# A planner's model of the opening's DMA loads is refitted, and with it the order of every engine's work

## What is computed

```python
out_d = sm_attn(q_d, k_d, v_d)                # q, k, v averaged over groups of 4 tokens
out_up = np.repeat(out_d, 4, axis=2)
mask = np.abs(pos[:, None] - pos[None, :]) < 4
scores = np.where(mask, scale * q @ k.T, -1e9)
out_local = softmax(scores) @ v
x = (out_up + out_local) as [tokens, 512]
h = x @ w_in;  g = s * relu(h)**2 + b;  x = g @ w_out      # layer 1
h = x @ w_in2; g = h - tanh(h);         out = g @ w_out2   # layer 2
```

## Time and profile before

| what | us |
|---|---|
| median of 3 runs | 893.32 |
| lowest, highest | 892.18, 893.84 |
| the profiled execution | 892.53 |
| its span | 890.7 |
| TensorE busy in the span | 876.7 |
| VectorE, ScalarE, GpSimd busy | 592.2, 467.4, 362.7 |

### The profile page before, as it was taken

How to read it: one execution, slowest core, us unless ns; L and a number is a source line. 1 busy time by engine, 2 the same in 40 slices (tenths; PEclk the granted TensorE clock), 3 DMA queues, 4 the chain that set the end, 5 groups by cost and what they waited for, 6 DMA issues and landing times.

```text
span 890.7 us, 15923 instructions
## 1 busy us (share of the span) xinstructions
PE 876.7 (98%) x5956; PEld 824.6 (93%) x5956; DVE 592.2 (66%) x799; ACT 467.4 (52%) x1144; POOL 362.7 (41%) x348
## 2 busy tenths in 40 slices
PE   7999999999999999999999999999999999999997
PEld 6889999999999999999999998988899888998896
DVE  5658599989999999985213377677734447444444
ACT  2899575567545754545565454444533336333332
POOL 5567473966489663433732100022221315212120
PEclk8999999999999999999999999999999999999999
DMA  8971453353333323202102250110601001310012
GB/s 219 277 247 46 120 147 85 106 128 94 97 94 88 88 46 72 71 1 79 56 28 65 80 181 24 27 45 25 189 25 44 29 24 48 95 43 29 24 49 71
DMA packets 57904, 73.57 MB, mean 83 GB/s; under 512 B 19110, under 2 KB 36068, under 8 KB 57828
## 3 DMA queue, kind: packets, MB, share of 16 engines
q1 hardware_dynamic: 56233, 72.12, 29.3%
q10 hardware_dynamic: 1595, 0.43, 0.2%
HBM read 63.10 MB, written 9.44 MB: 81 GB/s over the span
## 4 chain that ended last, share of the span: by engine, by line
PE 92%; DVE 3%; ACT 2%; DMA 1%; issue 1%; SPq 1%; POOL 0%; ACTq 0%; DVEq 0%; POOLq 0%
PE acc L2226 23%; PE hid L2198 22%; PE hid L2263 19%; PE acc L2280 14%; PE pa L2280 7%; PE pa L2156 1%; PE pa L2123 1%; PE pa L1998 1%; DMA dkey<-in_k_dram 1%; PE pa L2140 1%; DVE x2l L1610 1%; PE pa L2169 1%; PE acc L1990 1%; DVE sum L1655 0%; PE hid L2206 0%
## 5 line engine op out<-in xcount | busy, mean ns | idle before, releaser
L1248 POOL TENSOR_TENSOR gl<-relu,gh 128x288 fp32r<-128x288 f32 x128 | 128.3, 1005 | 171.1 <-PE acc L2226 119.5
L2226 PE MATMUL acc<-gh,wbh 128*128 128x288 f32 (+1 forms) x512 | 154.5, 302 | 0.0
L2198 PE MATMUL hid<-xh,wah 128*128 128x288 f32 x512 | 153.5, 301 | 0.3 <-ACT relu L1886 0.2
L2226 PE MATMUL acc<-gl,wbh 128*128 128x288 f32 (+1 forms) x512 | 151.5, 296 | 0.0
L2226 PE MATMUL acc<-gh,wbl 128*128 128x288 f32 (+1 forms) x512 | 151.2, 295 | 0.0
L2198 PE MATMUL hid<-xh,wal 128*128 128x288 f32 x512 | 150.4, 295 | 0.0
L2198 PE MATMUL hid<-xl,wah 128*128 128x288 f32 x484 | 142.0, 294 | 0.0
L1886 ACT ACTIVATE relu<-hid 128x288 f32<-128x288 f32 x128 | 52.3, 408 | 129.9 <-PE hid L2198 107.6
L2263 PE MATMUL hid<-x2h,wqh 128*128 128x384 f32 x336 | 113.2, 337 | 2.4 <-DVE odd L1646 2.4
L2263 PE MATMUL hid<-x2h,wql 128*128 128x384 f32 x336 | 113.2, 337 | 0.0
L2263 PE MATMUL hid<-x2l,wqh 128*128 128x384 f32 x336 | 112.8, 336 | 0.0
(11 more groups left out here) (210 smaller groups left out, 1863.7 us busy)
## 6 DMA issues: line engine op xcount, KB each, us to landing
w2b_raw<-in_moe_w_out_dram SPq DMA_DIRECT2D x24, 512.0 KB, 3.6
kl<-in_k_dram SPq DMA_DIRECT2D x23, 240.0 KB
vl<-in_v_dram SPq DMA_DIRECT2D x23, 240.0 KB
x2T<-ystage SPq DMA_DIRECT2D x8, 576.0 KB, 3.2
own<-in_q_dram SPq DMA_DIRECT2D x11, 384.0 KB
wa_raw<-in_moe_w_in_dram SPq DMA_DIRECT2D x4, 1024.0 KB, 8.8
wb_raw<-in_moe_w_out_dram SPq DMA_DIRECT2D x4, 1024.0 KB, 10.4
x2raw<-x2T SPq DMA_DIRECT2D x10, 384.0 KB, 3.9
```

Source lines behind the costliest of these rows:

```text
L1248: g.tensor_tensor(out=gl[:, turn % LRING1, 0:NS], in0=relu[:, f % 2, :], in1=gh[:, turn % GRING1, 0:NS].bitcast(F32), op=ALU.subtract).the ...
L2198: one = pe.matmul(dst, w[:, group, d, cols], x[:, j % XRING, d, :], start=i == 0, stop=i == 3 * KT - 1)
L2226: one = pe.matmul(acc[:, d, n], w[:, f, cols], g[:, turn % ring, n], start=(f == 0 and p == 0), stop=(f == FT - 1 and p == 2))
```

## The change

Only the planner's model of loads is edited. The modelled pipe is free at 2.0 us instead of 0; data counts as landed 1.5 us after the load leaves the pipe instead of 0.6, for every load of the program; and the sizes of the opening's loads are new. All orders, and the counts of fillers, follow from it. No instruction of the computation, no buffer and no wait is edited.

```diff
+FIRST_PACKET, LANDING = 2.0, 1.5
-        dma_free, emptied, held = 0.0, [0.0, 0.0], set()
+        dma_free, emptied, held = FIRST_PACKET, [0.0, 0.0], set()
                 dma_free = max(dma_free, start + 1.4) + kbytes / 230.0
-                end = dma_free + 0.6
+                end = dma_free + LANDING
-            o.add("SP", 0.6, (2, 2 * g + 3 * i), (kind, g), after, kbytes=620)
+            o.add("SP", 0.6, (2, 2 * g + 3 * i), (kind, g), after, kbytes=690)
-        o.add("SP", 1.6, (0, 0, half, 6), ("load_dense_keys", half), kbytes=330)
-    o.add("ACT", 2.5, (0, 0), ("load_first_queries",), kbytes=330)
-    o.add("SP", 1.6, (0, 0, 1, 6, 1), ("load_last_queries",), kbytes=330)
-    o.add("SP", 3.0, (1, 0, 0), ("load_dense_values",), kbytes=870)
+        o.add("SP", 1.6, (0, 0, half, 6), ("load_dense_keys", half), kbytes=360)
+    o.add("ACT", 2.5, (0, 0), ("load_first_queries",), kbytes=360)
+    o.add("SP", 1.6, (0, 0, 1, 6, 1), ("load_last_queries",), kbytes=360)
+    o.add("SP", 3.0, (1, 0, 0), ("load_dense_values",), kbytes=850)
-    for i, (kind, kbytes) in enumerate((("load_late_keys", 600), ("load_late_queries", 590), ("load_late_values", 870))):
+    for i, (kind, kbytes) in enumerate((("load_late_keys", 730), ("load_late_queries", 730), ("load_late_values", 850))):
-                  kbytes=(240 if b else 200) if n < 6 else 180)
+                  kbytes=(240 if b else 300) if n < 6 else 175)
```

## The result

The changed kernel takes 894.83 us (median of 19 runs, 892.68 to 896.21), the kernel before 892.84 (19 runs, 892.12 to 894.0). The ratio is 1.0019, 95% interval 1.0011 to 1.0026: slower by 0.19%, or 1.7 us (the medians themselves lie 2.0 apart). That is inside the 0.2% which the prediction called no change, but its sign is against the forecast of 891.1, and the interval holds no gain. Its runs also spread over 3.5 us, where those of before, taken with them, spread over 1.9; but 27 runs of the kernel before, taken later with other kernels, spread over 3.8. The profiled execution is 894.57 us, its span 892.8.

A forecast was written before the change was run, and what follows sets the result against it. ScalarE was taken to pace the opening behind the gate, TensorE the rest. Span 890.7 - 2.2 = 888.5, plus 1.8 gives 890.3, plus 0.8 for the median 891.1 us; range 888.9 to 895.3.

The forecast's parts named there:

- What bounds the kernel, and the gate: Opening: `dense_turn` 2 waits for loads until 17.33 us, unchanged; then ScalarE sets the pace to 43.31, TensorE bounds the rest.
- Whether the new model is nearer the trace: Opening's loads: old plan some 4 us early by the gate, new one within 0.7 us everywhere but 1.1 at the last.
- Fillers: TensorE ahead of the gate: 36 fillers for 24 move the first `dense_turn` from 7.5 to 8.1 us, costing nothing.
- VectorE: Opening: `dense_max` 0 goes ahead of the key sums; wins nothing by itself, may cost 0.5 us through `dense_keys` 2.
- ScalarE ahead of the gate: Three `place_columns`, from about 16 us, and `dense_exp` 1 move into ScalarE's idle time before 17.33: 2.73 us of work.
- The gain at `hidden1` (0, 0): End of the opening: 2.2 us sooner, at 41.1, between bounds of 1.7 and 2.73.
- The clock at the gate, priced at nothing: TensorE behind 17.33 us: full clock saves 2 to 3 us of its work, priced at nothing because ScalarE sets the pace.
- The failed step: Behind `hidden1` (0, 0): ScalarE's order nearly unchanged, reshuffles of batches 1 to 3 priced at 0, bounds -1.0 and +2.4 us.
- `load_w1b` 0 lands at 41.6, its first split comes at 42.5, nothing stands.: ScalarE behind `hidden1` (0, 0): weights needed at most 2.2 us sooner still land before their first use, so no wait.
- The slower one: 43 to 100 us: ScalarE bounds, four weight splits ahead of one `activate1` cost 2.1 us, twice 4.2; 895.3 us, chance 0.14.
- Lost on the way: Opening ends sooner, but later steps wait as much or ScalarE idles; gain 0 to 1.2, about 893 us, chance 0.23.
- the one for being wrong: Wrong if the gate moves, line 2198 starts as late as before, or the stretch behind `hidden1` grows by over 2 us.

The follow-up runs named there:

- the first experiment: Changed kernel with the modelled size of the eight w1 loads put back from 690 to 620: 890.29 us, 0.9975 of before.
- the run with the moved split: Kernel before with `w1_high` (0, 0) planned behind `score_exp` (0, 3): 892.05 us without added fillers, 891.36 with 26 more ahead of `dense_turn` 2.

## Why the prediction was wrong

The forecast was 891.1 and faster; the truth is 894.83 and slower by 0.19%.

- **What bounds the kernel, and the gate.** Right: loads stayed, the gate stayed, and nothing but the orders moved.
- **Whether the new model is nearer the trace.** Right, with one slip: the first value stage, planned at 22.2 and traced at 21.41, is 0.8 us off, not within 0.7.
- **Fillers.** The counts 36 and 28 are exact. The first `dense_turn` was to come at 8.1 and came at 7.22: the 36 took 5.78 us in all where 24 had taken 5.16. Their pace goes from some 0.21 us each to 0.12 on the way, and the moment varies from run to run: the same 24 fillers ended at 6.68 us in the kernel before and at 5.86 in the one with the gate filled, and with the same 36 the first `dense_turn` came at 8.27 in the kernel of the first experiment. The profile's granted clock is 1.00 for all of that time and does not show the step. The price of nothing was right: the gate waited for its loads all the same.
- **VectorE.** The order came as worked out. The feared half microsecond for `dense_keys` 2 did not arise: its copy was expected at 18.7 and ran at 18.03.
- **ScalarE ahead of the gate.** Right in mechanism and content (three `place_columns`, `dense_exp` 1), about 1 us sooner than forecast (14.89 against 16).
- **The gain at `hidden1` (0, 0).** 3.37 us, where 2.2 was taken with 2.73 as the upper bound. The stretch from `dense_queries` 2 got 24.68 - 21.67 = 3.0 us shorter (2.6 forecast), and it began 0.36 sooner. The mechanism was right: ScalarE's work there fell by 2.74 us (20.64 to 17.90), and its idle from 4.04 to 3.77. The bound of 2.73 left out the sooner start and the idle.
- **The clock at the gate, priced at nothing.** In the kernel before this is nearly right: full clock there alone moved `hidden1` (0, 0) by nothing and the time by 0.7 us, at the edge of the noise. In the new order the lower clock behind the gate goes with 1.1 us, and taking all fillers away costs 2.4. A price taken from one order was used in another.
- **The failed step: "its steps behind `hidden1` are the same and in nearly the same order, since their ranks decide", priced at 0 with bounds -1.0 and +2.4.** It cost 6.1 us, of which 4.5 are the late split with all that the plan puts in front of it and 1.6 the late load on top. I followed the plan only up to `hidden1` (0, 0), where it gave the right order, and put a phrase in place of the rest. Ranks decide only among steps that can start at the same time; in the plan `w1_high` (0, 1) is held back by the modelled landing of `load_w1b` 0 at 42.7, the splits behind it come later with it, and by then attention steps are ready that pass `w1_high` (4, 0). The kernels that move this one split show it in both directions (-4.5 and +4.1 us). The other part of the same pricing, a reshuffle of batches 1 to 3 at no cost, was right.
- **"`load_w1b` 0 lands at 41.6, its first split comes at 42.5, nothing stands."** Wrong too, since `hidden1` (0, 0) came 1.2 us sooner than forecast and the load 1.2 us later: the split came at about 40.5, the load landed at 42.75, ScalarE stood 2.24 us. Worth 0.7 to 1.9 us, by the measure taken.
- **The rivals.** The slower one had the right engine, the right stretch (43 to 100 us) and nearly the right time (895.3), but the wrong mechanism: splits set ahead of an `activate1`, at 2.1 us each. In truth splits were set too late, and two fifths of the cost, 2.5 us, are the clock, which it did not have. Its condition, over 4.0 us of new idle, was not met: it was 3.6. That its time came out so near is luck. "Lost on the way" (893) was too small and named no place. Of the signs set down, the one for being wrong decided: the stretch behind `hidden1` (0, 0) grew by over 2 us.

Why did a truer model of the loads make a slower order? By the planner's own count nothing was lost: it sees the new order and the one with the split back as equal to within 0.2 us at the end. It does count TensorE's idle around the late split, 5.9 us from `hidden1` (0, 0) up to 60 us against 2.5 with the split back. But in the order with the split back it counts 3.3 us more from 60 to 120 us, where that kernel's trace has 0.6. So it thinks the idle only moved. And it knows no clock, which is the other 2.5 us. What stays open is why the runs of the changed kernel spread over 3.5 us. The clock does not tell them apart: its mean over each run is 0.994 to 0.996 in all 19, 0.996 in the slowest and 0.995 in the fastest.

## What to carry to other kernels

When a planner's input changes, follow its orders past the point where the gain is booked, to the place where the next scarce engine is full, and look at which long steps of the bottleneck engine have moved behind short ones. A gain in the opening brings everything behind it forward against loads that have not moved, so list each load's landing and the new time of its first use before pricing the rest at nothing. Short waits close together can cost more than their sum: here two of 1.3 and 1.4 us with short steps between them were followed by 6.8 us of lower clock.

## What the runs showed of the hardware

- Behind two waits of 1.31 and 1.37 us with short steps between, TensorE went to 1.2 GHz for 6.8 us in the changed kernel, and again in the kernel before with the late split (0.67 from 60 to 70) and in the one with early load and late split. In the changed kernel without fillers, where the same two waits are 0.98 and 1.37, the low stretch lasted 3.4 us (60.2 to 63.6). Single idle times were followed by the same fall: 3.18 us at the gate in the kernel before and 2.39 us in the kernel with early load and late split (0.74 from 17.33 to 24). Filled to 1.11 us, the idle time at the gate of the kernel before was followed by none (1.00 from 17.33 to 24).
- A VectorE instruction that reads two SBUF tiles stands while GpSimd works on two SBUF tiles: a product takes 1.93 us beside GpSimd's subtraction against 0.51 with GpSimd idle. It happened again in the run with the moved split, where GpSimd made two low parts from 39.23 to 41.73; VectorE's and GpSimd's rows of that kernel:

```profile
40.91 1.13 DVE L1428 TENSOR_TENSOR xl<-xraw,xh 128x288 fp32r<-128x288 f32 x1 [0.64 <-ACT xh L1879]
```
```profile
39.23 2.50 POOL L1233 TENSOR_TENSOR wal<-wa_raw,wah 128x512 fp32r<-128x512 f32 x2 [7.25 <-ACT wah L1761]
```

  The usual duration of that row is 0.46. Started 0.82 us before GpSimd's end, it took about that much longer, less a little. The Trainium skill, "SBUF — State Buffer", section "Who interferes with whom", says that a VectorE instruction with two SBUF inputs contends with a GpSimd one that reads SBUF, and that the order of issue decides which of the two is blocked. On the contention the trace agrees, and VectorE, which started later, is the one that stood, here as in the kernel before (0.72 us, started inside GpSimd's 31.97 to 33.24). The order of issue does not explain all of the longest case: VectorE's product starts at 31.75, inside GpSimd's sum of 31.64 to 32.09, and GpSimd's next instruction, which starts only at 32.06, still goes first and keeps it standing to 33.32; it ends 0.36 later, at 33.68.
- The gate opened between 17.11 and 18.60 us in the profiled runs, with the same loads in the same order ahead of it (the earliest in the kernel without fillers, the latest in the one with early load and late split). Orders that hang on a landing must bear more than a microsecond of that.
